# Attention stage: the products of the global values take 64 rows per pair of heads, in four 64x64 parts of the TensorE array

## The chip, the cores and the metric

One core of one Trainium2 chip runs the whole kernel. The metric is the device time of one execution in microseconds. Before the change it is 627.2 us, the median of three runs (627.11 to 627.49).

## The reference

The kernel computes three layers one after the other: an attention with 32 global and 512 local tokens per sequence, a channel-mixing layer, and a layer with eight experts of which each token takes one. Only the attention is touched here:

```python
batch, n_heads, seq_l, seq_g, head_dim = (4, 8, 512, 32, 64)
s_g = scale * q_g @ all keys                      # the global queries see everything
out_g = softmax(s_g) @ all values
s_ll = q_l @ local keys, masked to |i - j| <= 32  # a local query sees 65 local keys
s_lg = q_l @ global keys                          # and the 32 global keys
out_l = softmax([s_lg, s_ll]) @ [v_g, v_l]
```

Everything is float32.

## The kernel before, in words

**Units.** The eight heads are taken as two "quads" of four heads. Of each batch and quad there are five units: four local units of 128 queries each, and then one unit for the 32 global queries. That makes 10 units per batch and 40 in all (`UNITS = 10`, `B = 4`). A quad has two pairs of heads; within a pair, head `h` (0 or 1) gives its results to PSUM partitions `64 h` to `64 h + 63`.

**One step.** Each engine runs through the same list of steps, and the order is written out by hand. In step `t` TensorE computes `scores(t)`, then `apply(t-2)`, then `turn(t-1)`:

- `scores` (L754 for local units, L768 for a global one) are the products of queries and keys. L754 uses operands of 64 rows and 64 columns, so its matmuls lie in four 64x64 parts of the array. L768 uses 128 rows and 64 columns.
- `apply` multiplies the turned probabilities by the values. For a local unit it first does the *global* values (L821, operand `vz`: 4 matmuls of 128 moving columns), and then the *local* ones (L830, operand `vw`: 8 matmuls of 64 moving columns). For a global unit it runs L845, L849 and L852. All of these use 128 (or 96) rows and 64 columns.
- `turn` transposes the probabilities with full 128x128 operands (L784 to L794), and last the tile `rb` (L798), which holds one over the sum of the probabilities.

A float32 matmul is recorded as two MATMUL and two LDWEIGHTS records, a transpose as one of each.

**What the other engines do in step t.** VectorE first masks the scores of unit `t` and takes their minimum, head by head (L1198; L1206 for a global unit, in one instruction). After the first head it adds a small number to the sums of unit `t-1` (L1217), after the second it takes their reciprocal (L1225). In step G, L1217 and L1225 come ahead of the mask instead. Then it multiplies the product of unit `t-2` into `xT` (`write_x`: L1247, L1244) and copies the first transposes of unit `t-1` out of PSUM (L1233, semaphore `probT_b`). ScalarE takes the exponentials (L1784) and copies the other transposes (L1794, `probT_a`). GpSimd spreads the reciprocals into the tile `rb` (L601; L599 for a global unit), for which L798 of TensorE waits (semaphore `spread`), and between units it rounds the weights of the next layer (L575, L579).

**The kinds of step.** By the unit whose scores are computed there are, in every five steps, one with global scores (step *G*, `t` = 4 or 9), the one after it (step *A*: it turns the global unit), the one after that (step *B*: it applies the global unit), and two steps in which all three units are local (steps *C*). L821 runs in steps G, A and C, not in B.

**The zeros in vz.** The operand `vz[:, k, :]` has 128 rows for each of the four heads `k`: the 32 rows of head `k` hold its global values, the other 96 are zero. The moving operand is the transpose of the probabilities of all four heads on the 32 global keys, 32 rows per head.

**PSUM.** `ps_o` is two banks. Before the change a unit has one of them, by the parity of its number: its columns 0 to 127 hold pair 0, and columns 128 to 255 pair 1.

Of the kernel before, what the change touches and what calls it, by code (L numbers as in the profile page):

```python
# [34 lines left out]
P = 128  # L35
B, H, SL, SG, DH = 4, 8, 512, 32, 64
# [4 lines left out]
QB = P // 2  # L41
HALO = 2 * WIN + QB
KW = HALO + SG
HEADS = 4
# [117 lines left out]
def program(nc, qk_t, qg_t, v_t, v_x, v_z, mu, w_9, w_9t, w_mix, w_e, out, x2_d):  # L162
    with ExitStack() as ctx:
# [569 lines left out]
        def _(pe):  # L733
# [67 lines left out]
            def apply(b, t):  # L801
                i, j = unit(t)
                n = UNITS * b + t
                o = ps_o[:, t % 2, :]

                def pt(k, first=0, n=P, rows=P):
                    c = P * (k if k < 2 else k + 2) + first
                    return probT[0:rows, t % 2, c:c + n]


                pe.wait_ge(probT_b, n + 1)

                if not (first_batch(b) and t < 2):
                    pe.wait_ge(x_written, n - 1)
                if j is not None:
                    pe.wait_ge(v_loaded[i][j], 16 * (b + 1))
                    if j == 0:
                        pe.wait_ge(vz_loaded[i], 16 * (b + 1))
                    for pair in range(2):
                        for h in range(2):  # L820
                            pe.matmul(o[DH * h:DH * (h + 1), P * pair:P * (pair + 1)], vz[i][:, 2 * pair + h, :],  # L821
                                      pt(HEADS), start=(pair == 0), stop=False)
                    for pair in (1, 0):
                        if pair == 0:
                            pe.wait_ge(probT_a, n + 1)
                        for blk in range(2):
                            for h in range(2):
                                k = 2 * pair + h
                                v0 = HEADS * DH * blk + DH * k
                                mm = pe.matmul(o[DH * h:DH * (h + 1), P * pair + QB * blk:P * pair + QB * (blk + 1)],  # L830
                                               vw[i][:, j, v0:v0 + DH], pt(k, QB * blk, QB), start=False, stop=(pair == 0 and blk == 1))
                else:
                    pe.wait_ge(vx_loaded[i], 16 * (b + 1))
                    rows = P - WIN
                    for cs in ((2, 3, 4), (0, 1)):
                        if cs[0] == 0:
                            pe.wait_ge(probT_a, n + 1)
                        for pair in range(2):
                            for c in cs:
                                for h in range(2):  # L840
                                    k = 2 * pair + h
                                    od = o[DH * h:DH * (h + 1), SG * pair:SG * (pair + 1)]
                                    v0 = HEADS * DH + DH * k
                                    if c < JT - 1:
                                        mm = pe.matmul(od, vw[i][:, c, v0:v0 + DH], pt(c, SG * k, SG),  # L845
                                                       start=(c == 2 and pair == 0),
                                                       stop=(c == 1 and pair == 1))
                                    elif c < JT:
                                        mm = pe.matmul(od, vw[i][0:rows, c, v0:v0 + DH], pt(c, SG * k, SG, rows),  # L849
                                                       start=False, stop=False)  # L850
                                    else:
                                        mm = pe.matmul(od, vx[i][:, DH * k:DH * (k + 1)], pt(c, SG * k, SG, rows),  # L852
                                                       start=False, stop=False)
                mm.then_inc(applied, 1)
# [320 lines left out]
        def _(dve):  # L1175
# [58 lines left out]

            def write_x(b, t):
                i, j = unit(t)
                o, sums = ps_o[:, t % 2, :], probT[:, t % 2, 2 * P:4 * P]
                x = xT[:, 2 * i:2 * i + 2, bass.ds(S * b + 1, SG) if j is None else bass.ds(S * b + 1 + SG + P * j, P)]
                dve.wait_ge(applied, UNITS * b + t + 1)
                if j is None:  # L1240
                    sums = sums[:, 0:P].rearrange("p (a h q) -> p a h q", a=2, h=2)
                    for h in range(2):
                        rows = slice(DH * h, DH * (h + 1))
                        ins = dve.tensor_tensor(x[rows], o[rows, 0:2 * SG].rearrange("p (a q) -> p a q", a=2),  # L1244
                                                sums[rows, :, h, :], ALU.mult)
                else:
                    ins = dve.tensor_tensor(x, o[:, 0:2 * P].rearrange("p (a q) -> p a q", a=2),  # L1247
                                            sums.rearrange("p (a q) -> p a q", a=2), ALU.mult)
                ins.then_inc(x_written, 1)

# [862 lines left out]
```

## Time and profile before

| | |
|---|---|
| median of three runs | 627.2 us |
| the profiled execution | 627.01 us |
| its span, from first to last instruction | 625.0 us |
| TensorE busy | 608.4 us, 97% |
| VectorE / ScalarE / GpSimd busy | 66% / 51% / 28% |
| attention stage | from about 7.6 us to 121.6 us |

TensorE is busy nearly all the time over the whole span. "Busy" there means that some matmul is in flight. A matmul record is longer than the time for which it keeps the array from the next one, because the matmuls are pipelined; so the distance between starts says more than the busy time.

### The profile page before, as it was taken

The page shows a single profiled execution, that of the slowest core. Times are in us where ns is not written, and L with a number is a line of the kernel's source. Part 1 is how long each engine was busy: PE and PEld are TensorE (multiplying, and loading weights), DVE is VectorE, ACT ScalarE, POOL GpSimd, SP SyncE. Part 2 cuts the span into 40 slices and gives each one's busy share as a digit, 9 for nine tenths or more (in the row PEclk, how much of TensorE's full clock was granted, in tenths as well). Part 3 has the DMA queues.
Part 4 walks back from the last instruction along what each step waited for, and adds up shares of the span by engine and source line. Part 5 has one row for each costly group of instructions (what it writes and reads, how often), then busy time and mean ns, then how long its engine had stood idle before and what let it go on. Part 6 is the DMA issues. An engine that isn't in the chain of part 4 may idle for free.

```text
span 625.0 us, 14720 instructions
## 1 busy us (share of the span) xinstructions
PE 608.4 (97%) x4493; PEld 506.4 (81%) x4494; DVE 410.3 (66%) x1164; ACT 321.1 (51%) x697; POOL 176.5 (28%) x241
## 2 busy tenths in 40 slices
PE   7999999999999999999999999999999999999994
PEld 6888888888788888889979878788788888888883
DVE  3777679754878797786979869948626336372621
ACT  4776779677416614632544853647516226261610
POOL 3555455600000000000000331575724412552240
PEclk9999999999999999999999999999999999999998
DMA  9987885002210010000004752887825513572000
GB/s 325 364 265 252 282 271 201 18 2 85 83 53 0 1 50 18 0 34 35 0 35 153 250 221 60 286 299 256 335 75 170 179 32 135 212 249 90 12 29 3
DMA packets 32935, 84.66 MB, mean 135 GB/s; under 512 B 4602, under 2 KB 7418, under 8 KB 32896
## 3 DMA queue, kind: packets, MB, share of 16 engines
q1 hardware_dynamic: 26816, 70.03, 32.1%
q0 software_dynamic: 3200, 8.92, 4.2%
q10 hardware_dynamic: 2880, 5.24, 2.6%
q8 instruction: 19, 0.31, 0.2%
q14 instruction: 20, 0.16, 0.1%
HBM read 76.04 MB, written 9.70 MB: 137 GB/s over the span
## 4 chain that ended last, share of the span: by engine, by line
PE 86%; DVE 8%; ACT 2%; issue 2%; POOL 1%; DVEq 0%; POOLq 0%; ACTq 0%
PE banks L878 22%; PE banks L880 22%; PE banks L879 22%; PE banks L754 3%; PE banks L1068 3%; PE banks L821 2%; DVE we_lo L1520 2%; PE banks L830 2%; PE banks L784 2%; PE banks L768 1%; PE banks L987 1%; PE banks L798 1%; PE banks L794 1%; PE banks L860 1%; PE banks L845 1%
## 5 line engine op out<-in xcount | busy, mean ns | idle before, releaser
L1487 DVE CUSTOM_DVE_ANT_0 product<-x,xT 128x512 f32<-128x512 f32 x120 | 77.8, 687 | 0.5 <-DMA xT<-in_w 0.4
L1784 ACT ACTIVATE prob<-neg,negmax 128x160 f32<-128x160 f32 (+1 forms) x136 | 59.1, 436 | 29.6 <-DVE negmax L1198 20.0
L1762 DVE TENSOR_SCALAR hid<-banks 128x512 f32<-128x512 f32 x34 | 23.5, 691 | 72.7 <-PE banks L880 71.6
L1891 ACT ACTIVATE k_sum<-banks 128x512 f32<-128x512 f32 (+2 forms) x40 | 21.4, 534 | 91.0 <-PE banks L880 86.3
L878 PE MATMUL banks<-we_hi,hid_hi 128*128 (+1 forms) x160 | 66.6, 416 | 0.2 <-DVE hid_lo L1595 0.2
L878 PE MATMUL banks<-we_hi,xg_hi 128*128 (+1 forms) x160 | 64.6, 404 | 1.3 <-DVE we_lo L1520 1.3
L685 POOL MEMSET xg<- 128x1024 f32 x1 | 1.0, 954 | 220.9 <-ACT k_raw L1884 220.9
L880 PE MATMUL banks<-we_hi,hid_lo 128*128 (+1 forms) x160 | 62.7, 392 | 0.0
L880 PE MATMUL banks<-we_hi,xg_lo 128*128 (+1 forms) x160 | 62.6, 391 | 0.0
L879 PE MATMUL banks<-we_lo,hid_hi 128*128 (+1 forms) x160 | 62.5, 391 | 0.0
L879 PE MATMUL banks<-we_lo,xg_hi 128*128 (+1 forms) x160 | 62.4, 390 | 0.0
L878 PE MATMUL banks<-mix_hi,wk_hi 128*128 128x512 f32 (+2 forms) x160 | 57.4, 359 | 0.2 <-POOL wr_lo L579 0.2
L880 PE MATMUL banks<-mix_hi,wk_lo 128*128 128x512 f32 (+2 forms) x160 | 57.1, 357 | 0.0
L879 PE MATMUL banks<-mix_lo,wk_hi 128*128 128x512 f32 (+2 forms) x160 | 57.1, 357 | 0.0
L647 POOL TENSOR_TENSOR we_lo<-raw_end,we_hi 128x1024 f32 (+1 forms) x16 | 44.5, 2804 | 41.9 <-ACT we_hi L1871 32.4
L878 PE MATMUL banks<-wv_hi,k_hi 128*128 128x512 f32 x136 | 54.0, 397 | 1.3 <-DVE x L1547 1.3
L1198 DVE CUSTOM_DVE_ANT_0 neg<-banks,mask 128x160 f32<-128x160 f32 x128 | 37.7, 315 | 26.1 <-PE banks L754 24.9
L1943 ACT ACTIVATE hid_hi<-banks 128x512 fp32r<-128x512 f32 x40 | 24.0, 600 | 59.3 <-PE banks L1068 42.7
L879 PE MATMUL banks<-wv_lo,k_hi 128*128 128x512 f32 x136 | 53.0, 390 | 0.0
L880 PE MATMUL banks<-wv_hi,k_lo 128*128 128x512 f32 x136 | 53.0, 390 | 0.0
L679 POOL DMA_INDIRECT out_rows<-y,rows_out x20 | 26.5, 1323 | 78.5 <-ACT y L1999 65.1
L1595 DVE TENSOR_TENSOR hid_lo<-banks,hid_hi 128x512 fp32r<-128x512 f32 x40 | 27.6, 689 | 30.3 <-ACT hid_hi L1943 29.3
(294 smaller groups left out, 1488.1 us busy)
## 6 DMA issues: line engine op xcount, KB each, us to landing
xT<-in_w_e SPq DMA_DIRECT2D x36, 512.0 KB, 5.0
raw_end<-in_w_e SPq DMA_DIRECT2D x36, 512.0 KB, 5.1
qk<-in_qk_t SPq DMA_DIRECT2D x32, 448.0 KB, 6.4
vw<-in_v_t SPq DMA_DIRECT2D x32, 256.0 KB, 5.2
w_raw<-in_w_mix ACTq DMA_DIRECT2D x20, 256.0 KB, 4.6
x_rows<-x SPq DMA_DIRECT2D x17, 256.0 KB, 2.0
xT<-in_w SPq DMA_DIRECT2D x8, 256.0 KB, 3.3
vz<-in_v_z SPq DMA_DIRECT2D x8, 128.0 KB, 3.6
```

The source lines that it names most:

```text
L647: return pool.tensor_tensor(we_lo[:, buf, 2 * j:2 * j + 2, :].rearrange("p x a b -> p x (a b)"), raw_part(j).unsqueeze(1), we_hi[:, buf, 2 ...
L679: pool.indirect_dma_start(out=out[:, :], in_=y[:, b, :], in_offset=None, out_offset=bass.IndirectOffsetOnAxis(ap=rows_out[b][:], axis=0), ...
L878: pe.matmul(dst, left[0], right[0], start=first, stop=False)
L879: pe.matmul(dst, left[0], right[1], start=False, stop=False)
L880: return pe.matmul(dst, left[1], right[0], start=False, stop=last)
L1198: dve.tensor_tensor_reduce(neg[:, KW * k:KW * (k + 1)], s[:, h, KW * pair:KW * (pair + 1)], mask[:, m, :], -SCALE, HUGE, ALU.add, ALU.min, ...
L1487: dve.tensor_tensor_reduce(product[:, k % 2, :], x2[:, t, :], w9(e), 1.0, 0.0, ALU.mult, ALU.add, dot[:, t % 2, e:e + 1]).then_inc(dotted, 1)
L1595: dve.tensor_tensor(hid_lo[:, D * h:D * (h + 1)], ps_ht[:, h, :], hid_hi[:, D * h:D * (h + 1)].bitcast(F32), ALU.subtract).then_inc(hid_lo ...
L1762: dve.tensor_scalar(hid[:, D * h:D * (h + 1)], ps_h[:, h, :], 0.0, None, ALU.max).then_inc(hid_ready, 1)
L1784: act.activation(prob[:, t % 2, c], neg[:, c], ACT.Exp, scale=-1.0, bias=negmax[:, t % 2, k:k + 1], accum_out=rsum[:, t % 2, k:k + 1]).the ...
L1891: act.activation(k_sum[:, f % 2, 0:w], ps_k[:, f % 2, 0:w], ACT.Relu).then_inc(k_copied, 1)
L1943: act.activation(hid_hi[:, D * h:D * (h + 1)], ps_ht[:, h, :], ACT.Copy).then_inc(hid_hi_ready, 1)
```

## The change

In `apply` of a local unit each of the four matmuls of the global values takes only the 64 rows that belong to its pair of heads (rows 0 to 63 for heads 0 and 1, rows 64 to 127 for heads 2 and 3). With 64 output partitions per head, the four matmuls lie in the four different 64x64 parts of the array. The moving columns (128), the number of matmuls and what they add up to are as before. The other 64 rows of each operand were zero.

So that the two row halves of the array do not write to one PSUM bank, the results now lie by pair: bank 0 of `ps_o` holds pair 0 and bank 1 pair 1, and the parity of the unit chooses the columns within both banks. The first matmul in each bank and head opens the sum (`start=True`) for both pairs. One instruction `pe.sem_inc(stepped, 1)` is added in front of the four matmuls, and `write_x` reads its operand from the two banks.

```diff
@@ apply
-                o = ps_o[:, t % 2, :]
+                o = ps_o[:, :, P * (t % 2):P * (t % 2 + 1)]
...
+                    pe.sem_inc(stepped, 1)
                     for pair in range(2):
+                        rows = slice(2 * SG * pair, 2 * SG * (pair + 1))
                         for h in range(2):
-                            pe.matmul(o[DH * h:DH * (h + 1), P * pair:P * (pair + 1)], vz[i][:, 2 * pair + h, :],
-                                      pt(HEADS), start=(pair == 0), stop=False)
+                            pe.matmul(o[DH * h:DH * (h + 1), pair, :], vz[i][rows, 2 * pair + h, :], pt(HEADS)[rows],
+                                      start=True, stop=False)
...
-                                mm = pe.matmul(o[DH * h:DH * (h + 1), P * pair + QB * blk:P * pair + QB * (blk + 1)],
-                                               vw[i][:, j, v0:v0 + DH], pt(k, QB * blk, QB), start=False, stop=(pair == 0 and blk == 1))
+                                mm = pe.matmul(o[DH * h:DH * (h + 1), pair, QB * blk:QB * (blk + 1)],
+                                               vw[i][:, j, v0:v0 + DH], pt(k, QB * blk, QB), start=False, stop=(blk == 1))
...
-                                    od = o[DH * h:DH * (h + 1), SG * pair:SG * (pair + 1)]
+                                    od = o[DH * h:DH * (h + 1), pair, 0:SG]
...
-                                                       start=(c == 2 and pair == 0),
-                                                       stop=(c == 1 and pair == 1))
+                                                       start=(c == 2), stop=(c == 1))
@@ write_x
-                o, sums = ps_o[:, t % 2, :], probT[:, t % 2, 2 * P:4 * P]
+                o, sums = ps_o[:, :, P * (t % 2):P * (t % 2 + 1)], probT[:, t % 2, 2 * P:4 * P]
...
-                        ins = dve.tensor_tensor(x[rows], o[rows, 0:2 * SG].rearrange("p (a q) -> p a q", a=2),
+                        ins = dve.tensor_tensor(x[rows], o[rows, :, 0:SG],
                                                 sums[rows, :, h, :], ALU.mult)
...
-                    ins = dve.tensor_tensor(x, o[:, 0:2 * P].rearrange("p (a q) -> p a q", a=2),
+                    ins = dve.tensor_tensor(x, o,
                                             sums.rearrange("p (a q) -> p a q", a=2), ALU.mult)
```

## Rows read from the trace of the kernel before

**Rows 1.** The page, part 1: busy time, share of the span, instructions
```profile
PE 608.4 (97%) x4493; PEld 506.4 (81%) x4494; DVE 410.3 (66%) x1164; ACT 321.1 (51%) x697; POOL 176.5 (28%) x241
```
**Rows 2.** Busy time by stretch: PE, PEld, DVE, ACT, POOL, clock, DMA
```profile
80.00:94.00 14.00, 14.00 (x266) 11.84 (x262) 10.25 (x56) 10.40 (x40) 7.31 (x14) 1.00 0.79 259
```
**Rows 3.** Groups by line and shape, PE, 0 to 215 us
```profile
L754 PE MATMUL banks<-qk 64*64 64x160 f32 x512 | 24.6, 308 | 0.0
```
**Rows 4.** Chain of waits, 79.5 to 91.2 us: start, us, what
```profile
82.57 0.70 PE banks L754 x16
83.27 0.59 PE banks L821 x8
83.86 0.46 PE banks L830 x16
84.32 0.37 PE banks L784 x2
84.69 0.11 PE banks L786
...
85.29 0.70 PE banks L754 x16
...
88.01 1.23 PE banks L768 x24
89.24 0.47 PE banks L821 x8
89.70 0.47 PE banks L830 x16
```
**Rows 5.** Timeline of the weight loads (PEld): start, us, line, tiles, count
```profile
23.31 0.14 PEld L798 LDWEIGHTS banks<-ident,rb 128*128 128x128 f32 x1
...
79.06 0.25 PEld L794 LDWEIGHTS banks<-ident,prob 128*128 128x128 f32 x2
79.28 0.14 PEld L798 LDWEIGHTS banks<-ident,rb 128*128 128x128 f32 x1
...
80.29 0.20 PEld L845 LDWEIGHTS banks<-probT,vw 128*64 128x64 f32 x4 [0.23 <-DVE probT L1233]
...
82.49 0.48 PEld L754 LDWEIGHTS banks<-qk 64*64 64x64 f32 x16 [0.17 <-issue]
...
84.53 0.25 PEld L794 LDWEIGHTS banks<-ident,prob 128*128 128x128 f32 x2
84.84 0.20 PEld L798 LDWEIGHTS banks<-ident,rb 128*128 128x128 f32 x2
```
**Rows 6.** Timeline of GpSimd, the copies into rb
```profile
22.86 0.29 POOL L599 COPY rb<-rinv 128x128 f32<-128x128 f32 x1 [2.22 <-DVE rinv L1225]
...
78.91 0.29 POOL L599 COPY rb<-rinv 128x128 f32<-128x128 f32 x1 [2.28 <-DVE rinv L1225]
...
84.39 0.40 POOL L601 COPY rb<-rinv 128x256 f32<-128x256 f32 x1 [1.03 <-DVE rinv L1225]
```
**Rows 7.** Timeline of VectorE, 76.9 to 85.1 us
```profile
79.57 0.55 DVE L1233 COPY probT<-banks 128x384 f32<-128x384 f32 x1
...
83.59 0.33 DVE L1198 CUSTOM_DVE_ANT_0 neg<-banks,mask 128x160 f32<-128x160 f32 x1 [0.73 <-PE banks L754]
...
83.84 0.16 DVE L1217 TENSOR_TENSOR rsum<-rsum,eps 128x4 f32<-128x4 f32 x1
...
84.15 0.17 DVE L1225 RECIPROCAL rinv<-rsum 128x4 f32<-128x4 f32 x1
```
**Rows 8.** Chain of waits, 101 to 122 us
```profile
104.93 0.56 DVE probT L1233
...
119.93 0.30 POOL rb L599
120.23 1.24 POOL wr_lo L579
...
121.61 0.47 PE banks L878
```

## The prediction

> **What bounds the kernel now.** Start with the page's busy times [rows 1]: TensorE is busy 97% of the span, no other engine more than 66%. That would make every saved matmul worth its time. But busy time of pipelined matmuls is not a bound, so the second view is the busy time by stretch. In one quad of the attention [rows 2], 14.0 us for five steps, TensorE is busy 14.00 us, VectorE 11.84, ScalarE 10.25, at clock 1.00. VectorE is not full either, yet it stands in a chain with TensorE in each step, and in such a stage the latency of that chain can bound while all engines have idle time. The third view, the chain of waits [rows 4], runs through TensorE's rows alone. It doesn't settle the matter, because it merges small gaps into the instruction behind them. What settles it is the timeline of the weight loads (which show when TensorE really takes up a new operand) beside that of GpSimd.
>
> In a step A and in a step G the first load of L798 comes 0.22 us after the first load of L794 (79.06 to 79.28, [rows 5]): two transposes at 0.11 us, the free pace [rows 4]. In a step C the same distance is 0.31 us (84.53 to 84.84). L798 needs the tile rb. GpSimd's copy there ends at 84.39 + 0.40 = 84.79 [rows 6], 0.05 us before the load. So L798 in step C does not follow its predecessor, it follows rb. That holds in all 16 steps C: the load comes 0.05 us after the end of the copy every time, and the distance is 0.24 or 0.25 us in the first batch, 0.31 or 0.32 in the second and third, and 0.26 to 0.49 in the last. The rows shown are one of these.
>
> Where does rb get its time from? From the scores of the same step: L754 starts loading at 82.49 [rows 5], VectorE has waited 0.73 us for it when it starts the first mask at 83.59 [rows 7], then L1217 at 83.84, the second mask, L1225 at 84.15 to 84.32, GpSimd at 84.39 to 84.79, L798 at 84.84, and behind its two transposes the next scores. So a step C is this loop: 1.10 us from scores to mask, 0.80 from mask to GpSimd, 0.40 for the copy, 0.05, then 0.37 to the next scores, in all 2.72 us (82.57 to 85.29 in the chain, [rows 4]). The product of the values is not in it. It lies beside it, with L821 at 83.27 to 83.86 [rows 4].
>
> **The change part by part: the matmuls of the global values.** L821 is 8 records in a local unit. Where it follows L768, which uses the same part sizes, they take 0.47 us [rows 4]: four rounds of two, 0.117 each. Where it follows L754, in 64x64 parts, they take 0.59: the switch of part sizes costs 0.12. The switch from L830 to the transposes costs 0.37 - 2 x 0.11 = 0.15 [rows 4]. That four 64x64 parts run at once is to be seen in L754: its 16 records pass in 0.70 us, switch included [rows 4], though one lasts 308 ns on average [rows 3], and its 16 weight loads lie within 0.48 us [rows 5]. So the new L821 takes two rounds, 0.235 us.
>
> *Steps C and A (L754, L821, L830).* Before: 0.59 + 0.46 = 1.05 us. After: 0.235 without a switch, for the parts are those of L754; then a switch of 0.12 to 0.15, and 0.46: 0.82 to 0.84. TensorE's own work becomes 0.22 us shorter.
>
> *Steps G (L768, L821, L830).* Before: 0.47 + 0.47 = 0.94 us, no switch. After: a switch, 0.235, a switch back, 0.46: 0.94 to 1.00. Here TensorE's work becomes 0.00 to 0.06 us longer. The change between 128x64 and 64x64 parts in this direction is in no row. From below it could be free, 0.12 less per step; I take the nearest row, L754 to L821, and a cost of 0.05.
> The Trainium skill (TensorEngine Tiling (Array Packing), Key Properties) says that changing the tiling mode drains the engine, while going from tile to tile in one mode does not. That speaks against this change in step G: by it both switches are paid, which is the 0.05 that I took from the rows; without it step G would gain 0.07 us and the sum would be 0.8 us lower.
>
> **What lies on the path.** *16 steps C: nothing is gained.* TensorE comes to L798 0.22 us sooner and waits 0.22 us longer for rb (0.31 in the step shown, where it waits 0.09 already). Behind L798 stand the next scores, which is what the loop is made of. VectorE's write_x and L1233 come behind four masks, so they don't start sooner either.
>
> *Seven steps A that count:* L798 loads at 79.28; rb is there at 78.91 + 0.29 = 79.20 [rows 5, 6]; with the 0.05 us from copy to load it could come at 79.25. So 0.03 us is to be had, not 0.22. In the first batch it is 23.31 against 22.86 + 0.29 + 0.05 = 23.20, 0.11 us. The seven give 0.00 to 0.11 each, 0.3 us together. Some is lost at once: in the step B behind it, L845 has waited for VectorE's copy L1233 (79.57 + 0.55 = 80.12, load at 80.29, [rows 5, 7]), and that copy hangs on the scores of step A. I count 0.15 us of gain.
>
> *Seven steps G:* rb is early there (L1217 and L1225 come ahead of the mask), all is at TensorE's pace, so the 0.05 counts in full: 7 x 0.05 = 0.35 us. The eighth step G, that of the last unit, counts nothing: the mixing layer starts at 121.61 behind GpSimd's last rounding (120.23, 1.24 us), which comes behind rb of the last unit (119.93) [rows 8] and so behind its scores, not behind L821.
>
> *The last batch.* From 104.93 on the chain goes through VectorE [rows 8], which has the first inputs of the next layer to make there. L821 in it is off the path, and the small gain of its step A is gone; that is in the 0.15 above.
>
> **The smaller edits.** The added `sem_inc` is one more instruction on TensorE's queue ahead of L821, behind the waits for probT_b, x_written and the loads; behind it stand L821, L830 and the turn. The queue handles such instructions while the array works on L754, so it costs 0; were it not hidden, it would cost at most 0.23 us, the idle time that weight loads wait before L821 or L845 [rows 5], and in steps C even that lies within the wait for rb. The new place of the results costs write_x nothing: equal elements, and the next unit's products wait for probT_b, which VectorE gives behind write_x, so nobody writes into the two banks during the read. The two `start` flags cost nothing.
>
> **The sum.** +0.35 - 0.15 = +0.2 us. The profiled execution took 627.0 (span 625.0 and 2.0 around it), so 627.2; the median of the runs is 0.2 above it, so 627.4. With all bounds: from -0.8 - 0.3 (free switch, all of A) to +0.06 x 7 + 0 = +0.4, that is 626.1 to 627.6, and run to run some 0.2 on each side.
>
> **The rivals.** *TensorE's pace is the bound (5%).* If rows 1 are taken at their word, 16 steps C and 8 steps A gain 0.22 each, 5.3 us, less 0.35: 622.2. For it speaks that the chain of waits names TensorE's rows only; against it the 0.05 us between copy and load in all 16 steps C.
>
> *The loop itself gets shorter (6%).* Today the array is drained behind L754; if the signal of the scores then leaves about 0.1 us sooner or later when L821 follows without a switch, 16 steps C move by that: sooner is 1.6 us, 625.8. The row for it is the 1.10 us from the first load of L754 to the mask, of which 0.70 is matmuls, so 0.4 us are open to such an effect. Against it: nothing shows that this time depends on what follows.
>
> *Slower: the four parts run two by two (8%).* Place: L821 itself, where two parts share the moving rows and two the output columns. Then it takes 0.47 us as today. Steps C and A stay as they are (0.47 plus one switch instead of one switch plus 0.47), but steps G pay two switches, 0.24 to 0.30 us, in full: 7 x 0.27 = 1.9 us, 629.1. It decides the sign from 0.2 us per step G on ((1.25 + 0.15) / 7). Against it L754, whose parts share rows and columns in just this manner.
> The Trainium skill (TensorE: Matmul & The Clock Gate, Part 3, The mechanism) says that a weight load overlaps with matmuls in flight only if it goes to other rows of the array. By it the two parts that share rows would load one after the other and this rival would come out. This trace does not agree: 16 loads of L754, of 0.13 us each, pass in 0.48 us.
>
> *The change does not change the pace of L821 (5%)*, for instance because the weight loads take the time: same sum as the forecast within 0.3 us.
>
> **How the numbers follow.** The forecast has 76%. A measurement of this kernel tells a change from none at about 0.2%, 1.25 us. Forecast and last rival lie within that (81%, of which I leave 2% for unknown causes on either side); the first two rivals make it faster, the third slower. So: faster 0.13, same 0.78, slower 0.09. For 8 in 10 the range takes the forecast with its bounds and goes part of the way to the second and third rival: 626.1 to 628.4.
>
> **What would show it right or wrong.** L821 in a step C: 8 records in about 0.24 us behind L754, no idle time ahead, and 0.12 to 0.15 ahead of L830. L794 to L798: the distance becomes 0.5 us in steps C, L798 still 0.05 us behind GpSimd's copy, and its wait for rb now among the longest of TensorE, some 16 x 0.3 us. Steps C still 2.72 us from scores to scores, G some 0.05 longer, A at most 0.03 shorter (0.11 in the first batch). The mixing layer starts at 121.6 to 122.0. Wrong would be: steps C shorter than 2.65, or steps G longer by more than 0.1.

## The result: 2.9 us slower, and the profile after

| | before | changed |
|---|---|---|
| median of the runs side by side | 627.13 us | 630.05 us |
| lowest to highest (20 runs each) | 626.17 to 628.95 | 627.34 to 632.4 |
| ratio, 95% interval | | 1.0046 [1.0034, 1.0059] |
| the profiled execution / its span | 627.01 / 625.0 | 627.34 / 625.4 |

The prediction, 627.4 us with a range to 628.4, was wrong. Note the last row before any trace is read: the profiled execution of the changed kernel is the fastest of its 20 runs. Its trace shows what the change does to the steps when TensorE is never held up, and that is nearly what was forecast: its span is 0.4 us longer. The 2.9 us are in the other executions.

The page, part 1, hardly moves (answers to [rows 1]), and part 3 lists a queue that the prediction leaves out, though the page of before has the same line (columns: packets, MB, share):

```profile
PE 608.1 (97%) x4493; PEld 501.6 (80%) x4494; DVE 410.6 (66%) x1164; ACT 321.1 (51%) x697; POOL 173.4 (28%) x241
...
q8 instruction: 19, 0.31, 0.2%
```

The groups by line and shape of the changed kernel, 0 to 215 us: L823, the new global values, now has 64x64 operands, like L754 [rows 3].

```profile
L754 PE MATMUL banks<-qk 64*64 64x160 f32 x512 | 25.1, 313 | 0.0
...
L823 PE MATMUL banks<-probT,vz 64*64 64x128 f32 x256 | 13.8, 285 | 0.4 <-DVE probT L1234 0.3
```

A step C in the second pass of the loop: timeline of the weight loads (answers to [rows 5]), and of GpSimd (to [rows 6]):

```profile
54.83 0.48 PEld L754 LDWEIGHTS banks<-qk 64*64 64x64 f32 x16 [0.17 <-issue]
55.30 0.28 PEld L823 LDWEIGHTS banks<-probT,vz 64*64 64x64 f32 x8
55.75 0.55 PEld L832 LDWEIGHTS banks<-probT,vw 128*64 128x64 f32 x16 [0.17 <-issue]
56.37 0.20 PEld L784 LDWEIGHTS banks<-ident,prob 128*128 128x128 f32 x2
56.65 0.25 PEld L794 LDWEIGHTS banks<-ident,prob 128*128 128x128 f32 x2
57.18 0.20 PEld L798 LDWEIGHTS banks<-ident,rb 128*128 128x128 f32 x2 [0.28 <-POOL rb L601]
57.55 0.48 PEld L754 LDWEIGHTS banks<-qk 64*64 64x64 f32 x16 [0.17 <-issue]
```
```profile
56.73 0.40 POOL L601 COPY rb<-rinv 128x256 f32<-128x256 f32 x1 [1.03 <-DVE rinv L1226]
```

From scores to scores it is 54.83 to 57.55, 2.72 us, the same as before ([rows 4]: 82.57 to 85.29). L823 follows L754 without a gap, the switch of part sizes now stands ahead of L832 (0.17 idle), L794 to L798 has become 0.53 us (it was 0.31), and L798 starts 0.05 us after the copy ends (56.73 + 0.40 = 57.13). The 0.22 us saved on TensorE stand idle in front of L798.

The chain of waits of the changed kernel (start, us, what), the step G that follows (answers to [rows 4]):

```profile
60.34 1.23 PE banks L768 x24
61.57 0.38 PE banks L823 x8
61.95 0.61 PE banks L832 x16
```

L823 and L832 take 0.99 us together, where L821 and L830 took 0.94.

### The profile page after: what moved, and what is told of

The parts are those of the page before. It is cut to its first block, busy times and chain, and to the rows that moved or that the text cites. A ratio compares the mean times of both kernels' runs of the same rounds, so it can differ in the third digit from the quotient of the medians.

```text
span 625.4 us, 14747 instructions
## 1 busy us (share of the span) xinstructions
PE 608.1 (97%) x4493; PEld 501.6 (80%) x4494; DVE 410.6 (66%) x1164; ACT 321.1 (51%) x697; POOL 173.4 (28%) x241
## 4 chain that ended last, share of the span: by engine, by line
PE 84%; DVE 9%; issue 3%; ACT 2%; POOL 1%; DVEq 0%; POOLq 0%; ACTq 0%
PE banks L879 22%; PE banks L881 22%; PE banks L880 22%; PE banks L754 3%; PE banks L1069 3%; DVE we_lo L1521 2%; PE banks L832 2%; PE banks L798 1%; PE banks L768 1%; DVE neg L1199 1%; PE banks L988 1%; PE banks L784 1%; PE banks L823 1%; DVE mix_raw L1460 1%; PE banks L794 1%
```

## Where the time is lost: TensorE's own code comes late

A second profile of the changed kernel is of a common execution (628.96 us, 1.95 above the profile of before).

> The changed kernel itself, again. Its steady steps cost what the forecast says (step G +0.07 us, steps C unchanged), which is 0.1 to 0.5 us in all, but its runs lie 3 us above the kernel before, between 627.3 and 632.4. Theory K (clock): TensorE waits 0.2 us longer for rb in 16 steps C, so it is less active in the attention and the clock is granted at half rate for some stretch in many runs; then the runs are 629 to 631 at the middle, the profile shows a stretch at 0.5 within the attention, and slower runs have a lower mean clock. Theory L (layout): the results in two PSUM banks cost something that comes and goes; then the trace shows longer matmuls or longer VectorE reads at clock 1.0. Theory D (transfers): a transfer that TensorE or another engine waits for lands late in some runs.

Ten runs: 629.61 us (628.41 to 631.76), ratio 1.0043 [1.0029, 1.0057]. Timeline of the weight loads of this execution, at two places:

```profile
33.90 0.14 PEld L832 LDWEIGHTS banks<-probT,vw 128*64 128x64 f32 x1
35.05 0.25 PEld L832 LDWEIGHTS banks<-probT,vw 128*64 128x64 f32 x5 [1.01 <-issue]
...
41.19 0.14 PEld L794 LDWEIGHTS banks<-ident,prob 128*128 128x128 f32 x1
42.20 0.14 PEld L794 LDWEIGHTS banks<-ident,prob 128*128 128x128 f32 x1 [0.87 <-issue]
```

TensorE stops for 1.01 and 0.87 us in the middle of one line, between two loads of the same group: no semaphore can be the cause, and the view has nothing but "issue". In the kernel before, the same place passes at once:

```profile
39.95 0.14 PEld L794 LDWEIGHTS banks<-ident,prob 128*128 128x128 f32 x1
40.06 0.25 PEld L798 LDWEIGHTS banks<-ident,rb 128*128 128x128 f32 x2
...
40.48 0.48 PEld L754 LDWEIGHTS banks<-qk 64*64 64x64 f32 x16 [0.17 <-issue]
```

Both stops together are 1.88 us. Set against before instruction by instruction, ScalarE's work in this execution falls back by 2.03 us between 30.7 and 45.6 us and by some 0.1 in the rest of the attention, so the stops are nearly the whole loss. The granted clock of this execution is 1.00 from 7.6 to 122 us, so it is not the clock.

What comes just before such a stop is seen in the DMA queues. Columns: packets, MB, share of 16 engines; 39.6 to 40.9 us of the same execution:

```profile
q8 instruction: 1, 0.02, 5.0%
```

One packet of 16,384 bytes lands at 40.76 us, and TensorE goes on at 42.20. Over the attention stage the stops of all traces but one (the kernel with shifted code, below) are at the same places of its queue, to within a few records (number 233, 365, 500, 635, 772, 907 and 1044, if weight loads, semaphore and branch records are counted), and always 1.3 to 1.6 us behind the landing of a q8 packet. With the matmuls counted too, one per load, the places are number 451, 707, 963, 1218, 1475, 1731 and 1986, that is 255 to 257 apart; 16,384 bytes over 256 records are 64 bytes for each. So I read the packets as TensorE's code, fetched in pieces of 256 instructions; the trace doesn't name the engine of the queue, but timing and spacing both fit. All the stops lie in the first batch and the first pass through the loop. The table gives, for the first four places, when the piece landed, when the first load behind it went, and the margin: that difference less 1.45. A margin of about 0 is a stop, or a piece that came only just in time; a larger one is a piece that was there in time. The place is known to a few records, so a margin is good to 0.1 us, and to 0.4 where a wait stands close by. Each row is one execution, and the first three rows show how much one can tell: the changed kernel has stops in one trace and none in the other.

```
                 place 233            place 365            place 500            place 635
before           17.61>21.06 +1.99    23.62>26.87 +1.80    30.04>33.81 +2.33    35.98>40.49 +3.06
changed          16.86>21.11 +2.80    23.65>27.17 +2.07    30.65>34.04 +1.94    35.39>40.13 +3.29
changed again    18.02>20.99 +1.51    24.21>27.05 +1.39    33.51>35.07 +0.11    40.76>42.20 -0.01
sem_inc alone    16.96>21.38 +2.97    24.70>27.59 +1.45    31.36>34.44 +1.62    36.58>40.58 +2.56
layout alone     16.95>21.84 +3.44    24.21>27.66 +2.00    30.32>34.60 +2.82    37.23>41.27 +2.59
64 rows, batch 0 20.14>21.62 +0.03    27.80>29.25 -0.00    34.27>36.12 +0.40    42.41>43.77 -0.10
64 rows, loop    16.88>21.40 +3.08    24.39>27.62 +1.78    30.89>34.46 +2.12    35.99>40.55 +3.11
64 rows, t 0,1   17.62>20.47 +1.40    24.25>26.69 +0.99    31.05>33.53 +1.03    35.29>39.67 +2.93
64 rows, t 5..7  17.49>20.28 +1.33    23.74>26.49 +1.30    32.01>33.42 -0.05    39.88>41.36 +0.03
loads 1 later    16.73>20.88 +2.70    22.65>26.94 +2.83    31.90>33.80 +0.45    37.52>39.89 +0.93
early sums, bef. 19.26>20.83 +0.12    25.61>27.04 -0.02    31.81>33.84 +0.58    39.54>41.14 +0.15
```

In the common execution the pieces are late, not TensorE early: the loads before a stop start no sooner than in before, while the landing at place 635 moves from 36.0 to 40.8 us. The data loads of the next batch, of which SyncE starts those of `qk` at 33.35 us, keep the DMA engines full there: their share is 0.99 from 34 to 40 us, and 0.91 in before.

The Trainium skill (Runtime: NRT & Kernel Launch, Instruction fetch mechanics) gives the same piece, a refill in blocks of 16 KiB (256 instructions) by the sequencer's own DMA queue. It says that the cost of crossing such a boundary is "mostly hidden". The packet size and the spacing of 255 to 257 records agree with it; the cost does not: 0.2 to 3.4 us per stop here.

## The experiments

Times beside each are medians; the kernel before, on the same chip, had 626.77 us beside the first four, 627.31 beside the two halves and the loads one unit later, 627.24 beside the lighter and the earlier-sum kernels, 627.43 beside the kernels with shifted code and with a few units, and 627.40 beside the loads two units later and the last kernel of all.

**One part at a time.** The `sem_inc` alone, in the kernel before:

```diff
+                    pe.sem_inc(stepped, 1)
                     for pair in range(2):
```

> The kernel before with the one sem_inc ahead of the products of the global values, nothing else. Theories K, L and D: 627.1, no change from before (within 0.5 us). If the added instruction on the queue is what costs, this is 629 to 631.

627.4 us (626.28 to 631.15, 12 runs), 1.0004 [0.999, 1.0018]. No cost to be told from none, as forecast; the interval still allows 1.1 us.

The two banks without the 64 rows, from the changed kernel:

```diff
-                    pe.sem_inc(stepped, 1)
...
-                            pe.matmul(o[DH * h:DH * (h + 1), pair, :], vz[i][rows, 2 * pair + h, :], pt(HEADS)[rows],
+                            pe.matmul(o[DH * h:DH * (h + 1), pair, :], vz[i][:, 2 * pair + h, :], pt(HEADS),
```

> The results lie by pair in two PSUM banks, but the products of the global values keep all 128 rows; no sem_inc. Theory K: 627.1 (within 0.5 us), since TensorE works as long as before. Theory L: 629 to 631, as the changed kernel.

627.11 us (12 runs), 1.0003 [0.9993, 1.0013]. No cost here either. Both edits together stand in the kernels below that have 64 rows only in the loop or only in units 0 and 1, and those lose nothing measurable (1.0008 and 1.0005). So between before and the changed kernel it is the 64-row products that bring the loss.

**Two transposes more in front of L798.** The changed kernel with useless work put where TensorE waits for rb:

```diff
+                if j in (1, 2):
+                    for _ in range(2):
+                        pe.transpose(ps_t[:, 0, 2 * P:3 * P], ident[:], ident[:])
                 pe.wait_ge(spread, n + 1)
```

> The changed kernel with two more 128x128 transposes of the identity ahead of L798 in every turn of local units 1 and 2 (16 in all), into the columns that L798 writes next: 0.22 us more of TensorE's work within the wait for rb of steps C. Theory K: the activity of before is back and costs nothing on the path, so 627 to 628 with little spread. Theories L and D: 629 to 631, as without them.

631.44 us (627.45 to 633.16, 10 runs), 1.0056 [1.0034, 1.0078]. Giving TensorE its work back does not bring the time back, so the theory that its longer waits cost it the clock (K) is out. Most steady steps keep their length (2.72 us in steps C; a few steps are 0.10 to 0.15 longer), but this median is above the changed kernel's, and the profiled execution (632.17) has one long stop. Its timeline of the weight loads:

```profile
39.16 0.55 PEld L850 LDWEIGHTS banks<-probT,vw 128*64 128x64 f32 x14
43.12 0.19 PEld L850 LDWEIGHTS banks<-probT,vw 128*64 128x64 f32 x2 [3.41 <-issue]
```

Its DMA queues from 33 to 40.5 us have no piece of q8 at all; it comes between 40.6 and 41.7 (last row):

```profile
q1 hardware_dynamic: 637, 1.86, 74.4%
q10 hardware_dynamic: 157, 0.29, 15.1%
q14 instruction: 1, 0.01, 0.8%
...
q8 instruction: 1, 0.02, 5.7%
```

In the kernel before the same stretch holds one:

```profile
q1 hardware_dynamic: 599, 1.82, 66.7%
...
q8 instruction: 1, 0.02, 0.9%
```

**First batch or loop.** The first batch is written out by itself, the other three are passes through a loop. The 64 rows only in the first (and, in the other kernel, only in the loop):

```diff
-                        rows = slice(2 * SG * pair, 2 * SG * (pair + 1))
+                        rows = slice(2 * SG * pair, 2 * SG * (pair + 1)) if first_batch(b) else slice(0, P)
```

> The 64-row products only in the first batch (code that is written out, units 0 to 7); in the other three batches (the loop) the 128 rows. Results by pair in two banks and the sem_inc throughout. Theory C (code): what is lost is lost once, at 34 to 45 us, where TensorE stands still with no semaphore open, 1.4 us after the landing of a 16 KB piece of its own instructions; the loss is made in the first batch and at the start of the first pass of the loop, and the later passes have their code already. Then this kernel is slow as the changed one: 628.5 to 631, with runs spread over some us. Theory P (pace): each 64-row step costs a bit; then this has a quarter of the 2.9 us, 627.8.

> The other half: 64-row products only in the loop over batches 1 to 3, 128 rows in the first batch. Theory C: mostly as the kernel before, 627 to 628; only the stall at the start of the loop (record 634 of TensorE's loads, at 40 us) can still come, since the 64-row steps ahead of it are few. Theory P: three quarters of the loss, 629.2.

First batch only: 629.61 us (628.61 to 632.1, 6 runs), 1.0042 [1.0026, 1.0058], the whole loss. Loop only: 627.57 (11 runs), 1.0008 [0.9999, 1.0017]. Timeline of the weight loads of the former, three stops of 3.47 us together:

```profile
21.62 0.14 PEld L798 LDWEIGHTS banks<-ident,rb 128*128 128x128 f32 x1 [0.57 <-issue]
...
29.25 0.19 PEld L754 LDWEIGHTS banks<-qk 64*64 64x64 f32 x2 [1.54 <-issue]
...
43.77 0.14 PEld L794 LDWEIGHTS banks<-ident,prob 128*128 128x128 f32 x1 [1.36 <-issue]
```

A term of the steady steps would have shown in the loop, with 24 of the 32 local units. It is in the 8 of the first batch.

**Which units.** In the first batch only, the 64 rows for units 0 and 1, or for 5, 6 and 7:

```diff
-                        rows = slice(2 * SG * pair, 2 * SG * (pair + 1))
+                        rows = slice(2 * SG * pair, 2 * SG * (pair + 1)) if first_batch(b) and t in (0, 1) else slice(0, P)
```

> 64-row products in units 0 and 1 of the first batch only (steps 2 and 3, ahead of the first boundary or on it), 128 rows elsewhere. If what decides is the first piece of code, asked for at about 12.5 us behind the first loads: slow, 628.5 to 630. If the later units matter: 627.3.

> 64-row products in units 5 to 7 of the first batch only (steps 7 to 9). The counterpart: slow, 628.5 to 630, if the pieces needed at 34 and 40.5 us decide; 627.3 if the first does.

Units 0 and 1: 627.29 us (12 runs), 1.0005 [0.9994, 1.0016]. Units 5 to 7: 628.82 (12 runs), 1.0021 [1.0008, 1.0035], 1.4 us, with this stop at place 635:

```profile
39.53 0.14 PEld L794 LDWEIGHTS banks<-ident,prob 128*128 128x128 f32 x1
41.36 0.14 PEld L794 LDWEIGHTS banks<-ident,prob 128*128 128x128 f32 x1 [1.69 <-issue]
```

About half of the loss comes with three units (1.4 of 2.9 us, by the medians).

**The place of the data loads.** SyncE starts the loads of the next batch when a unit's scores and products are done. One unit later, in the changed kernel and in the one before; two units later (`+ 7`), in the changed one:

```diff
-                    sp.wait_ge(scored, UNITS * (b - 1) + 5 * i + 5)
+                    sp.wait_ge(scored, UNITS * (b - 1) + 5 * i + 6)
...
-                    sp.wait_ge(applied, UNITS * (b - 1) + 5 * i + 5)
+                    sp.wait_ge(applied, UNITS * (b - 1) + 5 * i + 6)
```

> The changed kernel, with SyncE starting each load of scores and of values for the next batch one unit (2.7 us) later; nothing else. In the traces so far the boundaries between 16 KB pieces of TensorE's code are crossed at 20.0, 26.7, 33.8, 40.5 and 47.2 us, and the loads for the next batch begin at 19.3, 25.7, 33.2, 39.7 and 47.3, each time 0.5 to 1 us ahead of them. Theory C: a piece of code asked for then stands behind 1.1 to 1.8 MB of data; with the loads 2.7 us later it goes ahead of them, and the runs come down to 627 to 627.5 with a small spread. Theory P: 630 as before.

> The kernel before with the same later loads. Theory C: as before or a little faster, 626.2 to 627, without the runs above 628. Theory P: no change, 626.8.

> The changed kernel with every load for the next batch started two units (5.4 us) later; one unit gave 627.6, with 3 of 11 runs at 634 to 636. If it is the place of a load against the time at which the next piece of TensorE's code is asked for, two units bring the start of a load about 2 us ahead of the next boundary (31.1 against 33.8, 38.6 against 40.5), and the piece meets the full load again: 629 or more. If it is only that later loads leave more room, it is 627.6 or less.

One later, changed kernel: 627.59 us, but 11 runs in two groups, eight at 626.76 to 628.16 and three at 634.35 to 635.62; 1.004 [1.0008, 1.0072]. The eight lie 1.9 us and more under the changed kernel's median, the three are not explained, and with them the ratio is no better than the changed kernel's. One later, before: 627.16 (11 runs), 1.0001 [0.9993, 1.001]. Two later, changed: 629.26 (626.84 to 633.07, 12 runs), 1.003 [1.0014, 1.0045], with stops of 0.32, 0.55, 0.62 and 1.23 us at places 635 to 1044. The trace with the loads one unit later (of an execution of 626.97 us) has no stop. So the stops move with the data loads though no instruction of TensorE is touched; but that is one trace each, and a smaller loss on average is not shown.

**Less data in the second batch.** The loads of `qk` and `vw` that run during the first batch bring 16 partitions instead of 128, so batch 1 computes with old data:

```diff
+                    m = P if b != 1 else 16
-                    sp.dma_start(qk[i][:, j, :], qk_t[row + P * j:row + P * (j + 1)]).then_inc(qk_loaded[i][j], 16)
+                    sp.dma_start(qk[i][0:m, j, :], qk_t[row + P * j:row + P * j + m]).then_inc(qk_loaded[i][j], 16)
```

> The changed kernel with light traffic: of the queries, keys and values of batch 1 SyncE loads 16 partitions of 128 (so batch 1 is computed with old data in the others). 5.6 MB less between 19 and 42 us; every instruction of every engine stays. Theory C (a piece of TensorE's code comes late behind data): the stalls at records 364, 500 and 634 are gone, time 0.3 to 0.5 us above the same cut of the kernel before, where it was 2.9. Theory P: 2.9 above it, whatever the traffic.

> The kernel before with the same light traffic. Both theories: 626 to 627; under C its spread of some us becomes less too. It is what the light changed kernel is compared with.

Changed: 640.12 us (5 runs), before: 639.41 (5 runs). Both are 12 us longer, nearly all of it behind the attention (the page has 4553 matmuls instead of 4493; I take it that the tokens of batch 1 then go to other experts). So only their difference can be read: 0.7 us, where the two kernels with their full loads are 2.8 or 2.9 apart. Set against the kernel beside them they have 1.0207 [1.0187, 1.0227] and 1.0192 [1.0174, 1.0209], so these two are not told apart; by their five runs each, a difference over some 1.8 us is unlikely (an estimate). Neither trace has a stop, every margin is 0.96 or more, and from first to last scores the lighter changed kernel takes 108.54 us, as before (108.48). With little data in the way the pieces come in time.

**Code moved along by 32 instructions.** To shift the places of the pieces, in both kernels, ahead of the first turn:

```diff
+                    for _ in range(32):
+                        pe.sem_inc(stepped, 1)
```

> The changed kernel with 32 sem_incs more on TensorE's queue ahead of the first turn of all, where TensorE waits 2 us for the first exponentials. They take no time of the path; they move every later boundary between 16 KB pieces of TensorE's code 32 instructions of 256 earlier, some 0.85 us, against the loads of SyncE. Theory C1 (it is where a boundary falls against the loads that decides): the runs leave 629.6, to either side; down to 627.3 if a piece is now asked for ahead of the loads. Theory C2 (it is how long TensorE takes for a piece of code in the first batch): no change, 629 to 631.

> The kernel before with the same 32 sem_incs. C1: its time moves too, up to 628 to 630 if it now has the bad place. C2: 627.

Changed: 632.63 us (6 runs), 1.008 [1.0054, 1.0105]; before: 628.85 (12 runs), 1.0023 [1.0014, 1.0033]. For the time this is inconclusive, for the shift wasn't free. TensorE's timeline in the shifted before: the first turn waits 3.87 us, where before it waits 1.97 at 10.88:

```profile
13.17 0.41 PE L787 MATMUL banks<-ident,prob 128*128 128x128 f32 x2 [3.87 <-ACT prob L1787]
```

That all moved by 1.9 us, so places and loads both changed. The changed kernel has stops there (0.75 and 0.53 us) and the one before has none. But where they lie is the best evidence that the q8 packets are TensorE's code. Timeline of the weight loads of the shifted changed kernel:

```profile
35.66 0.19 PEld L826 LDWEIGHTS banks<-probT,vz 64*64 64x64 f32 x3
36.60 0.20 PEld L826 LDWEIGHTS banks<-probT,vz 64*64 64x64 f32 x5 [0.75 <-issue]
...
42.50 0.31 PEld L850 LDWEIGHTS banks<-probT,vw 128*64 128x64 f32 x6
43.34 0.42 PEld L850 LDWEIGHTS banks<-probT,vw 128*64 128x64 f32 x10 [0.53 <-issue]
```

Without the shift the stops of these two places come 16 and 14 loads later in the program, in the products of the local values and in a transpose (33.90 to 35.05 and 41.19 to 42.20 above). Counted with the matmuls and the 32 new records, though, they are number 963 and 1218 as before: the places stay where they were in the stream of instructions, and the program moved under them.

**Sums and reciprocals ahead of the masks.** If L798 waits for rb, then taking VectorE's L1218 and L1226 ahead of the mask in all steps, as step G does, should shorten steps C in both kernels, and more in the changed one:

```diff
-                if last and unit(t)[1] is None:
+                if last:
                     guard_sums(*last)
                     invert_sums(*last)
-                mask_scores(b, t, last)
+                mask_scores(b, t, None)
```

> The changed kernel, with VectorE taking the sums and reciprocals of unit t-1 ahead of the masks of unit t in every step, not only in steps G: VectorE is idle there for 0.7 us. Then rb is ready 0.8 us sooner and L798 no longer waits. If the wait for rb is what took the 0.22 us per step C and A, steps C shrink from 2.72 to 2.4 to 2.45 and the attention by some 4 us in its loop passes; the late code in the first batch stays or grows. So 624.5 to 627, against 630 now. If the array's work was not shortened, or something else takes the place of rb, steps C stay above 2.6 and it is 629 or more.

> The kernel before with the same order on VectorE. Only the 0.03 to 0.1 us that its steps C wait for rb can go: 1.0 to 1.5 us in all, 625.5 to 626.3, steps C 2.63. The difference to the changed kernel with this order is what the 64-row products are worth when nothing hides them.

Timeline of the weight loads of the changed kernel with this edit:

```profile
84.71 0.48 PEld L754 LDWEIGHTS banks<-qk 64*64 64x64 f32 x16 [0.17 <-issue]
85.34 0.24 PEld L823 LDWEIGHTS banks<-probT,vz 64*64 64x64 f32 x8 [0.15 <-issue]
...
86.64 0.25 PEld L794 LDWEIGHTS banks<-ident,prob 128*128 128x128 f32 x2
86.86 0.25 PEld L798 LDWEIGHTS banks<-ident,rb 128*128 128x128 f32 x2
87.28 0.48 PEld L754 LDWEIGHTS banks<-qk 64*64 64x64 f32 x16 [0.17 <-issue]
```

L794 to L798 is 0.22 us again, L798 no longer waits, the step is 2.57 us (the other steps C of the loop passes 2.45 to 2.65, and one 2.74) and a loop pass 27.29 instead of 28.03. The loop through rb is thus shown to be what swallowed the gain. The next limit is L823 itself, which starts at 85.34, 0.11 us behind the end of VectorE's copy for `probT_b` (84.67 + 0.56):

```profile
84.67 0.56 DVE L1234 COPY probT<-banks 128x384 f32<-128x384 f32 x1
```

Yet the time is 629.35 us (625.72 to 632.2, 12 runs), 1.0034 [1.0015, 1.0053]: the first batch has stops of 1.29, 1.35 and 2.19 us. The same edit in the kernel before gives 626.5 (625.7 to 628.65, 12 runs), 0.9993 [0.9982, 1.0004]. Its trace (627.34 us) is worth a line, for it has stops as well, without any 64-row product: 0.87, 0.27 and 0.81 us at places 233, 365 and 635, again 1.4 to 1.6 us behind a landing. The last of them:

```profile
41.14 0.48 PEld L754 LDWEIGHTS banks<-qk 64*64 64x64 f32 x16 [0.81 <-issue]
```

**Both only in the loop.** 64 rows and early sums where no piece should be late:

```diff
-                        rows = slice(2 * SG * pair, 2 * SG * (pair + 1))
+                        rows = slice(2 * SG * pair, 2 * SG * (pair + 1)) if not first_batch(b) else slice(0, P)
...
-                if last and unit(t)[1] is None:
+                if last and (unit(t)[1] is None or not first_batch(b)):
...
-                mask_scores(b, t, last)
+                mask_scores(b, t, last if first_batch(b) else None)
```

> A version put together from the runs so far: the first batch as in the kernel before (128 rows, sums and reciprocals behind the masks), and in the loop over batches 1 to 3 the 64-row products together with the sums and reciprocals ahead of the masks. In the trace of h_guard_after a pass of the loop takes 27.3 us against 28.0 before. If code is late only in the first batch, the three passes keep their gain: 2 us less the last batch's share, 625 to 626, faster than both kernels (about 627.3 and 629.8). If code comes late at the start of the loop too, 627 or more.

627.41 us (626.48 to 628.38, 11 runs), 1.0004 [0.9995, 1.0013]: no gain. Busy time by stretch (PE, PEld, DVE, ACT, POOL, clock, DMA share, GB/s), the second loop pass and the last batch, first of this kernel, then of before:

```profile
65.88:93.15 27.27, 27.19 (x517) 22.34 (x516) 21.69 (x111) 20.64 (x80) 15.16 (x28) 1.00 0.84 280
93.15:116.09 22.94, 22.22 (x417) 17.88 (x416) 22.11 (x100) 21.43 (x74) 12.92 (x23) 1.00 0.45 146
```
```profile
65.54:93.57 28.03, 28.03 (x517) 23.65 (x516) 20.42 (x111) 20.71 (x79) 14.86 (x29) 1.00 0.81 273
93.57:116.08 22.51, 22.43 (x417) 18.71 (x416) 21.40 (x101) 21.19 (x75) 13.54 (x24) 1.00 0.47 153
```

The second loop pass gains 0.76 us, and the last batch gives 0.43 back: VectorE is busy 22.11 of its 22.94 us and was the limit there already ([rows 8], 104.93). The first loop pass starts even and ends 0.34 us late (65.88 against 65.54), with stops at places 772, 907 and 1044, two of which are:

```profile
53.47 0.48 PEld L847 LDWEIGHTS banks<-probT,vw 128*64 128x64 f32 x13 [0.36 <-issue]
...
60.59 0.53 PEld L768 LDWEIGHTS banks<-qk,qg 128*64 128x64 f32 x10 [0.45 <-issue]
```

No version tried is clearly faster than the kernel before.

## Why the prediction was wrong, step by step

- *Four parts run at once.* Right: L823's 8 loads pass in 0.28 us without a switch (0.42 us for L821's, in the same place of before), and TensorE's turn begins 0.22 us sooner in steps C (1.54 us after the step's start instead of 1.76), the 0.22 that was worked out. The rivals "two by two" and "no change of pace" are out.
- *Steps C gain nothing.* Right: 2.72 us as before, rb's wait 0.28 us, load 0.05 us behind the copy; shown by the early sums, which take the wait away and shorten nearly every step C. TensorE's pace as the bound (622.2 us) is out, and so is a shorter loop.
- *Steps G +0.05.* Measured +0.065 (3.073 to 3.138). With the 0.235 us saved the two switches cost 0.30 us, so neither is free. The Trainium skill's rule that a change of mode drains the array (TensorEngine Tiling (Array Packing), Key Properties) agrees with that in this direction too, to which no row of before could speak.
- *Steps A.* Right in kind and too small: most go from 2.560 to 2.49 us, -0.07 each, where at most 0.03 was given, and the one in the first batch has -0.16 instead of 0.11. Two of the *steps B* behind them lengthen by 0.065, which I had not counted apart. From first to last scores the profiled execution has +0.13 us, leaving out one step in a stretch at half clock (below); the sum said +0.2. Its terms were off by more than their sum: that +0.13 is so close to +0.2 is in part luck.
- *The `sem_inc` and the two banks cost nothing.* Right as far as can be measured, each tried alone.
- *The sum and its bounds.* This failed. It took the steady steps for the whole, and "with all bounds" ended at +0.4, and the scatter at 0.2 on each side; the 20 runs of before alone go from 626.17 to 628.95. The missing term is the supply of TensorE's instructions in code that is passed for the first time: +1.88 us in one common execution, 2.9 in the median. It can't be had from matmul durations, since no instruction gets longer. The profile of before did show what it hangs on: 19 packets of "instruction" in a queue of their own, a DMA share of 0.79 in a quad [rows 2] and of 0.96 at 38 to 42 us (row below), and a margin of only some 1.3 to 3.3 us at the seven places of the pieces. Nothing on the page gives the margin; one has to lay the landings beside the loads. Busy time by stretch of the kernel before, where place 635 is passed:

```profile
38.00:42.00 4.00, 4.00 (x93) 3.32 (x85) 2.66 (x18) 2.92 (x12) 2.02 (x6) 1.00 0.96 341
```

- *The chances.* 0.13 and 0.78 and 0.09 are not quite what the text adds up to, which is 0.13, 0.77 and 0.10; nothing hangs on it.

**What stays open.** That the stops are late code in the first batch and the first loop pass is as good as shown: the spacing of 256 records, the places that stay in the stream when the program is shifted, the landing, the half (629.61 against 627.57) and the missing stops with little data. Why the 64-row products of three units make a piece land 2 to 4 us later is not. They are not the only thing that does: the early sums do it to the kernel before (landing at place 635 at 39.5 instead of 36.0 us), whose time is none the worse.

The trace has the landing of a piece and not its request. But in none of the 20 traces does a piece of the attention land before TensorE has passed the place ahead of it; it lands 0.85 to 7.96 us behind that. For places 500 and 635 this time is 2.8 and 2.2 us in before, 6.5 and 5.7 in the common execution of the changed kernel, and 1.2 and 2.6 in the lighter before. If a piece is asked for when the last one is entered, which fits but isn't shown, then the request goes out as early as ever and the piece is longer on its way beside the data. What in the changed order of work makes it so is open.

## What to carry to other kernels

Code that TensorE ran through for the first time was here a transfer like any other, and beside loads that filled the DMA engines it came late. So before a change in such a stretch is priced by durations, lay the "instruction" packets beside the timeline and see how much room each has. Work taken from an engine that waits for a loop through the others is worth nothing until that loop is shortened, and then the next limit may be near. A profile can be the luckiest of its runs: set its own time beside their median before concluding that nothing was lost.

## What the runs showed of the hardware that was not expected

- *TensorE can stop without a wait.* 0.2 to 3.4 us, marked only "issue", at places 255 to 257 records apart, ending 1.3 to 1.6 us behind a 16 KB packet of the instruction queue. Of the 19 packets of before 8 land by 61.7 us and the next at 127.1: the second loop pass and the last batch, which run the code of the first pass again, bring none.
- *A stop can cost more than itself.* After the stop of 3.41 us in the kernel with two more transposes, the granted clock was at the lower level, 1.2 GHz, from 44.4 to 47.8 us; ScalarE's work fell back by 5.3 us in all between 39 and 45.6. Busy time by stretch of that kernel, 38 to 46 us (the seventh number is the clock):

```profile
38.00:42.00 4.00, 1.75 (x53) 1.37 (x42) 1.46 (x11) 2.67 (x12) 1.93 (x5) 1.00 0.78 299
42.00:46.00 4.00, 2.86 (x33) 2.29 (x33) 1.05 (x4) 0.59 (x1) 0.29 (x1) 0.80 0.39 100
```

- *A stretch at half clock near the start.* The changed kernel's profile has it from 11.85 to 15.26 us and so do those of the layout alone, the `sem_inc` alone and the loop half, none of which is slower; their scores had begun earlier (6.70 us in the changed kernel's against 7.59 in before). That alone doesn't bring it: both kernels with early sums begin as early (6.86 and 6.78) and have none. One step took 3.99 us in it instead of 2.67:

```profile
11.80:15.30 3.50, 3.50 (x45) 3.03 (x45) 1.63 (x11) 2.50 (x12) 1.59 (x4) 0.51 1.05 387
```

- *Thirty-two `sem_inc` on TensorE's queue are not free.* The idle time ahead of the first turn was 3.87 us instead of 1.97, some 0.06 us each if all of it is theirs (an estimate), where the one per unit costs nothing measurable.
